# Later units' running maxima in two levels on their own rows, tiny TensorE products in place of long scans and moves, and transfers laid over 128 partitions

## What is computed

```python
for t in range(S):
    m_new = np.maximum(f_gate[:, :, t] + m, i_gate[:, :, t])
    f_stab = np.exp(f_gate[:, :, t] + m - m_new)
    i_stab = np.exp(i_gate[:, :, t] - m_new)
    m = m_new
    C = f_stab[:, :, None, None] * C + i_stab[:, :, None, None] * np.einsum('bhd,bhe->bhde', vt, kt)
    n = f_stab[:, :, None] * n + i_stab[:, :, None] * kt
    h_tilde = np.einsum('bhde,bhe->bhd', C, qt)
    denom = np.maximum(np.abs(np.einsum('bhd,bhd->bh', n, qt)[:, :, None]), 1.0)
    y[:, :, t] = h_tilde / denom / (1.0 + np.exp(-o_gate[:, :, t]))
# x is y with the heads side by side, p the normalised domain_probs
for e in range(E):
    out += p[:, e:e + 1] * (np.maximum(x @ w1[e], 0.0) @ w2[e])
```

## Time and profile before

| | before |
|---|---|
| median of 3 runs | 422.12 us (421.67 to 425.3) |
| the run that was profiled | 423.53 us |
| its span, first to last instruction | 421.8 us |
| PE busy | 412.9 us, 98% |
| DVE, ACT, POOL busy | 178.0, 166.0, 152.0 us |
| PE's granted clock, mean | 1.000 |
| transfers | 47.71 MB, mean 113 GB/s |

### The profile page before, as it was taken

How to read it: one execution, slowest core, us unless ns; L and a number is a source line. 1 busy time by engine, 2 the same in 40 slices (tenths; PEclk the granted TensorE clock), 3 DMA queues, 4 the chain that set the end, 5 groups by cost and what they waited for, 6 DMA issues and landing times.

```text
span 421.8 us, 6991 instructions
## 1 busy us (share of the span) xinstructions
PE 412.9 (98%) x2680; PEld 398.4 (94%) x2680; DVE 178.0 (42%) x364; ACT 166.0 (39%) x338; POOL 152.0 (36%) x188
## 2 busy tenths in 40 slices
PE   8799999899999999999999999999999999999997
PEld 8699989899999999999999999999999999999996
DVE  5684765655555556436233232323113123131142
ACT  6865679465253735424121441143211332111111
POOL 3566833793445855313010660056200355000000
PEclk9999999999999999999999999999999999999999
DMA  8889999599741677400000232013200010010010
GB/s 204 276 313 300 251 251 266 172 251 259 209 130 68 178 251 204 152 2 1 2 0 2 68 138 68 2 67 117 92 2 0 20 50 2 0 37 27 2 62 31
DMA packets 16868, 47.71 MB, mean 113 GB/s; under 512 B 2003, under 2 KB 8660, under 8 KB 15748
## 3 DMA queue, kind: packets, MB, share of 16 engines
q1 hardware_dynamic: 15972, 44.43, 36.0%
q10 hardware_dynamic: 864, 2.84, 1.9%
HBM read 45.18 MB, written 2.05 MB: 112 GB/s over the span
## 4 chain that ended last, share of the span: by engine, by line
PE 89%; DMA 4%; DVE 3%; ACT 1%; issue 1%; POOL 1%; SPq 1%; DVEq 0%; POOLq 0%; ACTq 0%
PE hid_ps L988 40%; PE acc_ps L1007 34%; PE out_ps L944 4%; PE score_ps L1007 3%; DMA w_raw<-in_w_b 3%; PE score_ps L903 2%; PE out_ps L951 2%; PE add_ps L924 1%; PE hid_ps L867 1%; DMA m_u<-y_acc 1%; PE acc_ps L988 1%; POOL w_lo L415 1%; ACT dec_w L510 1%; SPq L304 1%; DVE split_qk L688 0%
## 5 line engine op out<-in xcount | busy, mean ns | idle before, releaser
L747 DVE SCALAR_TENSOR_TENSOR h_lo<-hid_ps,h_hi 128x384 fp32r<-128x384 f32 (+2 forms) x120 | 67.9, 566 | 220.4 <-ACT h_hi L545 220.3
L545 ACT ACTIVATE h_hi<-hid_ps 128x384 fp32r<-128x384 f32 (+2 forms) x120 | 59.7, 497 | 233.5 <-PE hid_ps L988 233.0
L1007 PE MATMUL acc_ps<-w_hi,h_hi 128*128 128x320 f32 x352 | 110.3, 313 | 0.1
L1007 PE MATMUL acc_ps<-w_hi,h_lo 128*128 128x320 f32 x352 | 108.7, 309 | 0.0
L1007 PE MATMUL acc_ps<-w_lo,h_hi 128*128 128x320 f32 x352 | 108.4, 308 | 0.0
L988 PE MATMUL hid_ps<-xt_hi,w_hi 128*128 128x384 f32 (+2 forms) x360 | 104.1, 343 | 0.1
L988 PE MATMUL hid_ps<-xt_hi,w_lo 128*128 128x384 f32 (+2 forms) x360 | 103.8, 342 | 0.3 <-POOL w_lo L415 0.2
L415 POOL TENSOR_TENSOR w_lo<-w_raw,w_hi 128x384 fp32r<-128x384 f32 x56 | 59.8, 1071 | 114.3 <-ACT w_hi L531 114.3
L988 PEld LDWEIGHTS hid_ps<-xt_hi,w_lo 128*128 128x128 f32 x360 | 65.4, 188 | 4.8 <-POOL w_lo L415 0.7
L1007 PEld LDWEIGHTS acc_ps<-w_hi,h_hi 128*128 128x128 f32 x352 | 66.2, 188 | 1.6 <-DVE h_lo L747 0.3
L1007 PEld LDWEIGHTS acc_ps<-w_lo,h_hi 128*128 128x128 f32 x352 | 66.2, 188 | 1.3
(11 more groups left out here) (163 smaller groups left out, 368.3 us busy)
## 6 DMA issues: line engine op xcount, KB each, us to landing
w_raw<-in_w_b SPq DMA_DIRECT2D x25, 704.0 KB, 4.3
raw<-in_qk_s SPq DMA_DIRECT2D x8, 960.0 KB
g_all<-g_dram SPq DMA_DIRECT2D x10, 512.0 KB, 9.3
kv<-in_kv_n SPq DMA_DIRECT2D x12, 352.0 KB, 7.8
w_raw<-in_w_b ACTq DMA_DIRECT2D x3, 704.0 KB, 4.6
out_y<-y_acc SPq DMA_DIRECT2D x12, 160.0 KB, 1.8
carry<-g_dram SPq DMA_DIRECT2D x30, 60.0 KB
q_pack<-in_q_p SPq DMA_DIRECT2D x10, 180.0 KB, 9.6
```

Source lines behind the costliest of these rows:

```text
L545: nc.scalar.activation(h_hi[:, M % RING, 0:cols], hid_bank(M)[:, 0:cols], ACT.Relu).then_inc(hid_hi, 1)
L747: nc.vector.scalar_tensor_tensor(h_lo[:, M % RING, 0:cols], hid_bank(M)[:, 0:cols], 0.0, h_hi[:, M % RING, 0:cols].bitcast(fp32), ALU.max, ...
L1007: last = nc.tensor.matmul(acc_ps[t][:, 0:DM], x, w, start=(f == 0 and i == 0), stop=(f == NF - 1 and i == 2))
```

## The change

1. **Maxima in two levels.** `fi_rows` brings the gates of the first chunk only (16 x 2 x 128 in place of 16 x 2 x 768). `fi_units`, the gates of the 80 later rows, is now SP's second DMA. DVE scans all 80 rows at once from minus infinity (`local[:, 0]`) and sums their forget gates (`local[:, 1]`). PE carries the last column of both to the 16 rows by four products of 80 x 16 by 80 x 2 (`move_ends`), DVE makes the maxima at the chunk starts by one scan of 16 x 4 (`unit_starts`), PE carries them back by five products of 16 x 80 by 16 x 1 that add into one column (`move_starts`, with a shifted identity as weights), and one DVE instruction makes m of all 80 rows (`unit_maxima`). The scans of 256 and 384, the five DMAs and the wait on them are gone.
2. **Steps.** `unit_steps` gets both gate differences from one sum by a minimum and a maximum with 0. `gate_scan(1)` now stands ahead of `probs(1, 1)`.
3. **One function table.** The output gate is a Tanh of half the input, and `gate_x` adds 1 to it (`scalar_tensor_tensor` in place of `tensor_tensor`); the count column is 2.0 and the floor 2.0 to match. ACT's list holds 1 table load in place of 6.
4. **POOL.** `weigh_keys(0)` no longer waits for `gate_sums(1)`; `mask_heads` goes ahead of it.
5. **ACT.** The first weight pairs are issued earlier, the load of `y_acc[:, 2:4]` and `gate_open(2)` later: `gate_open(2)` now stands directly ahead of `relu(0)`, and blocks 2 and 3 are split behind `xt_high(1)`.
6. **SP.** `load_q(2)` and the scores of units 2 and 3 go ahead of the gate store, and weight pairs 3 and 4 behind unit 3's key-value load or its `carry`.
7. **One slot earlier:** `cast`, `subtract_high`, and `reload_scores` for units 5 and up.
8. **128 rows.** `raw` of units 4 to 11 and `q_pack` are loaded over 128 partitions in place of 120 (1024 KB and 192 KB in place of 960 and 180); what reads them still takes 120 rows.

```diff
-            for c in range(1, NC):
-                sp.wait_ge(m_half if c < 3 else m_ready, 1)
-                sp.dma_start(m_u[U0 * (c - 1):U0 * c, :], m_sb[:, L * c:L * (c + 1) + 1]).then_inc(m_moved, 16)
+            load_q(2)
+            reload_scores(2)
+            reload_scores(3)
             sp.wait_ge(gate_tiles[1]["ready"], 2)
...
-                if M == T0[3] + 5:
+                if M == T0[3] + 4:
                     reload_scores(5)
-                if (k := unit_at(M, -1)) is not None and NS <= k < NT - 2:
+                if (k := unit_at(M, -2)) is not None and NS <= k < NT - 2:
                     reload_scores(k + 2)
...
-            pool.wait_ge(gate_tiles[1]["ready"], 2)
+            mask_heads()
             weigh_keys(0)
             weigh_keys(1)
...
-                nc.scalar.activation(o, o, ACT.Sigmoid).then_inc(open_ready, 1)
+                nc.scalar.activation(o, o, ACT.Tanh, scale=0.5).then_inc(open_ready, 1)
...
-                if (k := unit_at(M, -5)) is not None and k >= NS:
+                if (k := unit_at(M, -6)) is not None and k >= NS:
                     cast(k, 0)
-                if (k := unit_at(M, -4)) is not None and k >= NS:
+                if (k := unit_at(M, -5)) is not None and k >= NS:
                     cast(k, 1)
...
+            def unit_steps():
+                gt = gate_tiles[1]
+                dve.wait_ge(m_ready, 1)
+                dve.wait_ge(local_ready, 3)
+                nc.vector.tensor_tensor(gt["fm"][:, :], gt["w"][:, :], m_u[:, :], ALU.add).then_inc(gt["step"], 1)
+                dve.wait_ge(gt["step"], 1)
+                nc.vector.tensor_scalar(gt["g"][:, :], gt["fm"][:, :], 0.0, None, ALU.min).then_inc(gt["step"], 1)
+                nc.vector.tensor_scalar(gt["j"][:, :], gt["fm"][:, :], 0.0, -1.0, ALU.max, ALU.mult).then_inc(gt["step"], 1)
...
+            def local_maxima():
+                dve.wait_ge(units_in, 16)
+                nc.vector.tensor_tensor_scan(local[:, 0, :], fi_u[:, 0, :], fi_u[:, 1, :], NEG, ALU.add, ALU.max)\
+                    .then_inc(local_ready, 1)
+                nc.vector.tensor_tensor_scan(local[:, 1, :], ones[0:U1, 0:L], fi_u[:, 0, :], 0.0, ALU.mult, ALU.add)\
+                    .then_inc(local_ready, 1)
+                nc.vector.tensor_tensor(gate_tiles[1]["w"][:, :], fi_u[:, 0, :], fi_u[:, 1, :], ALU.subtract).then_inc(local_ready, 1)
+            def unit_starts():
+                dve.wait_ge(ends_ps, 1)
+                ends = hid_ps[0][0:U0, 0:2 * (NC - 2)].rearrange("u (c t) -> u c t", t=2)
+                nc.vector.tensor_copy(end_sums, ends[:, :, 1]).then_inc(ends_set, 1)
+                dve.wait_ge(ends_set, 1)
+                nc.vector.tensor_tensor_scan(m_sb[:, L + 1:L + NC - 1], end_sums, ends[:, :, 0], m_sb[:, L:L + 1],
+                                             ALU.add, ALU.max).then_inc(starts_ready, 1)
+            def unit_maxima():
+                dve.wait_ge(starts_ps, 1)
+                nc.vector.tensor_copy(m_u[:, 0:1], hid_ps[0][0:U1, U0:U0 + 1]).then_inc(m_begun, 1)
+                dve.wait_ge(m_begun, 1)
+                dve.wait_ge(local_ready, 2)
+                nc.vector.scalar_tensor_tensor(m_u[:, 1:L], local[:, 1, 0:L - 1], m_u[:, 0:1], local[:, 0, 0:L - 1],
+                                               ALU.add, ALU.max).then_inc(m_ready, 1)
...
             probs(0, 0)
+            unit_maxima()
             probs(0, 1)
+            unit_steps()
             probs(1, 0)
-            dve.wait_ge(units_in, 16)
-            dve.wait_ge(m_moved, 16 * (NC - 1))
-            gate_steps(1, fi_u[:, 0, :], fi_u[:, 1, :], m_u[:, 0:L], m_u[:, 1:L + 1])
+            gate_scan(1)
             probs(1, 1)
             copy_keys(0, 0, U0, acc_ps[2])
-            gate_scan(1)
             gate_sums(1)
...
+                if (k := unit_at(M, -4)) is not None and k >= NS:
+                    subtract_high(k, 0)
                 if (k := unit_at(M, -3)) is not None and k >= NS:
-                    subtract_high(k, 0)
-                if (k := unit_at(M, -2)) is not None and k >= NS:
                     subtract_high(k, 1)
...
+            def move_ends():
+                pe.wait_ge(local_ready, 2)
+                for c in range(NC - 2):
+                    last = nc.tensor.matmul(hid_ps[0][0:U0, 2 * c:2 * c + 2], ident[0:U1, U0 * c:U0 * (c + 1)],
+                                            local[:, :, L - 1], start=True, stop=True)
+                last.then_inc(ends_ps, 1)
+            def move_starts():
+                pe.wait_ge(starts_ready, 1)
+                pe.wait_ge(shift_set, 2)
+                for c in range(NC - 1):
+                    at = U1 - U0 - U0 * c
+                    last = nc.tensor.matmul(hid_ps[0][0:U1, U0:U0 + 1], shift[:, at:at + U1], m_sb[:, L + c:L + c + 1],
+                                            start=(c == 0), stop=(c == NC - 2))
+                last.then_inc(starts_ps, 1)
...
+            move_ends()
             scores(0, 0)
+            move_starts()
             scores(0, 1)
```

121 lines of the change are left out of this document (56 added, 65 removed).

## The result

| | before | changed |
|---|---|---|
| median, 20 runs each | 422.5 us | 425.03 us (423.61 to 427.08) |
| ratio changed / before | | 1.0052, 95% interval 1.0037 to 1.0067 |
| the run that was profiled | 423.53 us | 423.94 us |
| its span | 421.8 us | 422.2 us |
| PE busy | 412.9 us | 414.4 us |

The change made the kernel slower by half a per cent, within the 1% that was called no change, and outside the forecast range of 417.0 to 420.6. The one that was profiled belongs to the shorter ones. (The expectations say 12 of 20; it is 11.)

What follows compares the result with a forecast made beforehand. PE, busy 98% of the span, was taken as the bound. Gains of 0.7 + 0.2 (a POOL wait at 32 us) + 0.95 + 1.7 = 3.55 us off 421.8 gave a 418.3 span, 418.6 us median; range 417.0 to 420.6.

Steps and rivals of the forecast that it cites:

- 0.3 below the median: Whole kernel: the profiled span, 421.8 us, was taken to stand 0.3 below the median of the runs, 422.12.
- A: `outputs(1)` at 16.19 us, waiting for `probs(1, 1)` and `copy_keys`: 1.66 us lost, 0.7 to be won (0 to 1.4).
- The tiny products: Eighteen PE instructions between the exponents and the second `scores`, wholly on the path: 18 x 0.07 = 1.26 us.
- it just fits: cost 0, cover 0.1: ACT's fuller list before `relu(0)`: `relu(0)` starts near 22.3, the low part is done at 23.4, `down(0)` at 23.5.
- Rival 4: Before `relu(0)`: `gate_open(2)` waits for its late load and PE loses time; at 25.2 all gains are gone; chance 0.05.
- SP and the transfers: Scores and `q_pack` fill the DMA hole at 14 us; the later weight pair lands near 50 instead of 55.6.
- C: At 56 to 58 us, `up(14)` held by a late weight pair: 1.27 us lost, 0.95 to be won (0 to 1.5).
- D: At 82 us, `scores(5, 0)` held by unit 5's second `subtract_high`: 1.68 us lost, 1.7 to be won.
- for units 6 to 11: The same shift moves 1.9 us of DVE work one slot earlier into DVE's idle time; PE has no wait to win.
- D's 1.7 is lost again when DVE or ACT meets PE a few slots on: Behind 82 us, one case of a wait taking another's place (chance 0.20 in all): 420.3 us.
- 128 rows: Loads of `raw` and `q_pack`: 0.6 MB or 2.7 us more transfer, spread over 200 us of mostly idle DMA: cost 0.
- The signs named as refuting: PE waits for `h_lo` in slot 0, or for `local_ready`, or PE's waits ahead of 100 us sum above 3.

Runs made afterwards that it cites:

- experiment 2: The changed kernel with the scores of units 2 and 3 issued behind the three gate stores instead of ahead of them: 422.25 us, ratio 1.0004.
- the repairs and unit 5 alone: Changed kernel: gate stores ahead of scores, `gate_open(2)` in slot 3, only unit 5's casts, subtractions and reload one slot earlier: 420.37 us, ratio 0.9951.
- unit 5 alone: The kernel before with only unit 5's casts, subtractions and reload one slot earlier: 420.99 us, ratio 0.9968.

## Why the prediction was wrong

- **Frame of the sum.** The run of that profile took 423.53, the medians of the kernel before are 422.1 to 422.8, so a span of 421.8 stands not "0.3 below the median" but belongs to an execution some 1.1 us longer than usual. Taken off the median of 422.1, 3.55 us still give 418.6; the sum was not wrong by this.
- **A, 0.7.** Right. The tiny products were forecast at 1.26; they take 0.28 + 0.80, and each group makes the product behind it start some 0.1 late (`scores` 1.06 and 0.97 from start to start in place of 0.92 and 0.86), 1.3 in all. From the first `scores` group's start to `outputs(1)` 7.52 us before; from the start of the tiny products 6.90 now: 0.62 won (0.8 to 1.1 against the other four profiles with the old gates, in which the wait at A is longer).
- **What the 0.7 met: "it just fits: cost 0, cover 0.1".** This step failed. DVE's `w_lo` takes 2.56 in place of 1.41 us beside POOL, which now splits at the same time, and the working does not list it; it costs 0.43 us from `up(0)` to `down(0)` (3.71 in place of 3.28), and still does where `gate_open(2)` is out of the way. And `gate_open(2)` waits 0.79 in the shorter execution and 4.56 in the longer one. `down(0)` starts at 24.25 and 26.70, before at 24.21. Cover of 0.1 us was no cover.
- **Rival 4, chance 0.05.** The mechanism was named, its rows too (the other load took 14.3 us); the size of the load was used as an argument against it. The load takes 8.9 and 11.7 us beside the scores, and at most 7.0 with the scores behind the stores (experiment 2), so the 832 KB beside it are a cause; what the 1.4 MB ahead of it on its own queue do was not tested. The chance was far too low.
- **SP and the transfers.** The step that cost most. It counted the scores that fill the hole at 14 us and what weight pairs gain later, and did not count what SP issues next, the gate store of 0.5 KB and the wait on it, with `g_all`, `carry` and pair 3 behind. It had been 3.45 us in flight (17.77 to 21.22) and became 6.4 to 9.5: 2.2 us of delay at the least for all three. This gives the 1.2 + 0.6 us at 33. In longer executions the same scores hold the load for `gate_open(2)` as well, which costs 3.9 us and a lower clock. One edit, the scores behind the store, brings the ratio from 1.0052 to 1.0004, and 3.8 us against two variants of the changed kernel in the same session (1.0092 and 1.0093).
- **C, 0.95.** Right, 0.88, with the rest of 0.24 on POOL as forecast. ACT is full there, as the working said, but what fills it is part 7's second cast: without part 7 all 1.6 us are won. And the moved transfers were not the only way to it: on the kernel before, part 7 alone takes the stretch to 4.43 as well (why the pair comes earlier then is not shown), the scores first alone to 3.75.
- **D, 1.7.** The wait on `split_qk` went, and 0.68 us of time. Of the 1.68 that the profile showed, 0.7 came from POOL holding the ports first. The forecast said that the same shift "for units 6 to 11" lies in DVE's idle time. It did not ask who runs beside DVE then. The rival "D's 1.7 is lost again when DVE or ACT meets PE a few slots on" was right in effect (0.95 given back), and partly in its reason: 0.57 by an ACT cast that makes DVE late, 0.38 by POOL blocked.
- **A slip of the sum.** Seven ACT operations at the pace of five in 3.2 us are 4.5 us, not 4.4; it changes nothing.
- **128 rows, one table, `gate_x`, POOL's order:** no cost found behind relu(6). POOL's new place is part of the collision at 21 us.
- The signs named as refuting were there: PE waits for `h_lo` in slot 0 behind `gate_open(2)`, and PE's inner waits are 3.6 us in sum.

What the gates in two levels bring by themselves is not settled. With the repairs and unit 5 alone the whole change gives 0.9951 (0.9933 to 0.9968), unit 5 alone on the kernel before 0.9968 (0.9947 to 0.9989). The intervals overlap. In the profiles relu(3) comes 0.7 to 0.9 us earlier (25.55 against 26.25 to 26.44), but most of that is that the exponents were done earlier in this execution: from their end to relu(3) it is 17.48 us, against 17.58 and 18.06 in the two profiles of before and 17.86 with unit 5 alone. That leaves 0.1 to 0.6 us for the gates and what stands with them. The 1.5 at C does not need the new gates: the scores moved alone, on the kernel before, give the same 3.75.

## What to carry to other kernels

When a large transfer is put into a hole of a queue, the first thing to price is the small one that is issued next on it, and all that waits for its landing; small stores that others depend on belong ahead of bulk, and the bulk then stands ahead of something else, which has to be priced too. A step of VectorE on two SBUF operands can make a GpSimd instruction beside it twice as long, or become longer by it, even in VectorE's idle time, so move as few of them as the wait asks for and ask who waits for either. And a wait that sits in the shadow of another one of the same cause shows its price only when the first is gone: repair the cause, not the waiter.

## What was not expected of the hardware

- A store of 0.5 KB took from 3.0 to 10.0 us to land: 5.3 to 10.0 with 832 KB ahead of it on its queue, 3.0 to 3.8 without, and once 7.2; with the same program 6.4 and 9.5 us in two executions.
- The granted clock fell to 1.2 GHz for 3 to 7 us behind idle times of PE of 3.85, of 3.79, of 3.30 and of 2.0 + 0.6 us, and once behind 1.76 us; it did not fall behind 1.2 + 0.6 us nor behind 1.96 us. It also fell with no idle time at all, behind 54 instructions of one or two columns.
- POOL's instructions of 0.87 to 1.01 us took 1.85 to 2.01 beside a subtraction of DVE on 40 rows of 1024 that had started first; where POOL started first, by 0.04 us, POOL's took 0.87 and the subtraction 1.90 in place of 1.21.
